# First MLP layer of an attention-MLP kernel: two of three token chunks by Strassen's algorithm in six of eight weight blocks

## The chip, the core and the metric

The kernel runs on one core of a Trainium2 chip. The metric is the device time of one execution in microseconds (us). Engines are called PE (TensorE matmul; PEld is its weight load), DVE (VectorE), ACT (ScalarE), POOL (GpSimd) and SP (SyncE, which here issues all DMAs). Each engine runs its own instruction stream in order; they meet only at semaphores.

## What is computed

The reference, cut to what matters here:

```python
x = attention(q, k, v, proj)        # 2 x 8 heads, 768 tokens, 64 wide -> x: 1536 x 512
h = x @ moe_w_in                    # 512 x 2048
r = np.maximum(h, 0.0)
g = s * (r * r) + b
y = g @ moe_w_out                   # 2048 x 512
a, c = y @ w1, y @ w2               # 512 x 1024 each
out = ((a * c) @ w3) @ w_out        # 1024 x 1024, 1024 x 512
```

All of it is float32. Each matmul factor is split into a high and a low part in a reduced format (`fp32r`), and a product is three matmuls: high by low, low by high, high by high.

## The kernel before, in words

Attention comes first; beside it `w3 @ w_out` is formed (`wc`). The stage that the change touches follows. Tokens are held transposed: `x_hi`, `x_lo` are 128 partitions x 4 row tiles (`KT`) x 1536 tokens, in three chunks of 512. The hidden width of 2048 goes in eight blocks (`fc`) of 256 = two tiles of 128. For a block and a chunk, PE forms two hidden tiles of 12 matmuls each (`hidden`, L1027, banks 0/1 or 2/3 in turn), and later four output tiles of 6 matmuls each (`out_of_hidden`, L1041, banks 4 to 7). PE takes the hidden tiles one chunk ahead of the outputs (`steps`, L1054). A waiting output product holds up all that stands behind it in PE's stream.

Between the two, ACT copies relu of the hidden tile out of PSUM (L637); DVE squares it with PSUM as the one operand (L847), scales it to `g_raw` (L851); ACT rounds it to `g_hi` (L643); DVE subtracts to `g_lo` (L855), and adds finished output tiles to `y_acc` (L867). DVE's order per step is: hidden work of the next chunk, then the four additions of this one (`steps`, L875).

Weights: SP loads 512 KB tiles into the two slots of `stage` (`load_w`, L253), and may issue tile w only when the low part of tile w-2 is done. ACT makes the high part (`w_high`, L556, in L558), POOL the low part (`w_low`, L406, in L408). A block has two tiles (`w_in`, `w_out`), in `w_c` or `w_b` by turns. The eight `w12` tiles of the next layer (`w1`, `w2`) go four into `w_a` in the first steps (`W12_A`), two into `w_c` in the last block and two into `w_b` behind the last output (`W12_B`, L681). The eight `wc_hi`/`wc_lo` splits (L630, L497) are made in steps 2 to 5 of the first six.

At the end `y_acc` is split for the next layer: ACT makes `x_hi` (L676), DVE `x_lo` (`y_low`, L869, in L873), chunk by chunk. The next layer (`second`, L1070) wants `x_lo` of chunk 0 to start; from its third unit of 24 matmuls on it also wants DVE's product `ab` (L896) of two units before, which needs ACT's copy `a_sb` (L690). In ACT's stream this copy stands behind the last `w12` high and the last `x_lo` (L683). Its last product with `wc` is L1095.

What orders the output products:

```python
def load_w(w, slot, src):
    after(sp, w_lo_done, w - 1)
...
pe.wait_ge(g_lo_done, 2 * n + 2)
for m in range(KT):
    after(pe, y_add_done, 4 * n + m - 3)
```

Of the kernel before, what the change touches and what calls it, by code (L numbers as in the profile page):

```python
# [41 lines left out]
def attention_mlp(nc, qk, v, proj, w_in, w_out, s, b, w12, w3t, w_out2, out):  # L42
    with ExitStack() as ctx:
# [171 lines left out]
        def _(sp):  # L215
# [291 lines left out]
        def _(act):  # L507
# [124 lines left out]
            def hidden(n, k):  # L632
                for f in range(2):

                    act.wait_ge(h_done, 2 * n + f + 1)
                    after(act, relu2_done, 2 * n + f - 1)
                    act.activation(relu[:, f], psum[:, 2 * (k % 2) + f, :], ACT.Relu).then_inc(relu_done, 1)  # L637
                for f in range(2):
# [4 lines left out]
                    act.activation(g_hi[:, k % 2, f], g_raw[:, f], ACT.Copy).then_inc(g_hi_done, 1)  # L643

            def steps(cp, first=False, last=False):
                for k in range(6):
                    hidden(6 * cp + k, k)
                    if k == 0:

                        after(act, y_mm_done, 24 * cp)  # L650
                        first_layer_weights(of_layer(2 * cp + 1), cp + 8 if first else 2 * cp + 10, 1)
                    if first and k in (1, 2):

                        for j in (2 * k - 2, 2 * k - 1):
                            w_high(W12_A + j, (W12_A + j) // 2 + 1, j % 2, high(w_a, j))
                    if first and k in (2, 3):
                        for i in range(4 * k - 8, 4 * k - 4):
                            wc_high(i)
                    if k == 3 and not last:
                        act.wait_ge(y_mm_done, 24 * cp + 12)  # L660
                        first_layer_weights(of_layer(2 * cp + 2), 2 * cp + 11, 0)
                    if k == 4 and last:
                        act.wait_ge(y_mm_done, 24 * cp + 12)
                        for j in range(2):
                            w_high(W12_B + j, W12_B // 2 + 1, j, high(w_c, j))
# [40 lines left out]
        def _(dve):  # L706
# [137 lines left out]
            def hidden(n, k):  # L844
                for f in range(2):
                    dve.wait_ge(relu_done, 2 * n + f + 1)
                    dve.scalar_tensor_tensor(relu2[:, f], psum[:, 2 * (k % 2) + f, :], 0.0, relu[:, f],  # L847
# [5 lines left out]
                for f in range(2):
                    dve.wait_ge(g_hi_done, 2 * n + f + 1)
                    dve.tensor_tensor(g_lo[:, k % 2, f], g_raw[:, f], g_hi[:, k % 2, f].bitcast(F32),  # L855
                                      ALU.subtract).then_inc(g_lo_done, 1)

            def add_y(n, t, first=False):
                for m in range(KT):
# [15 lines left out]
            def steps(cp, first=False, last=False):  # L875
                for k in range(6):
                    if not (last and k == 5):
                        hidden(6 * cp + k + 1, k + 1)
                    add_y(6 * cp + k, k % NCH, first=first and k < NCH)
                    if last and k == 4:  # L880
                        y_low(0)

            hidden(0, 0)
            steps(0, first=True)
# [19 lines left out]
        def _(pe):  # L904
# [149 lines left out]
            def steps(cp, last=False):  # L1054
                for k in range(6):
                    if not (last and k == 5):
                        hidden(6 * cp + k + 1, k + 1, 2 * cp + (k + 1) // NCH)
# [88 lines left out]
```

## Time and profile before

| what | value |
|---|---|
| median of 3 runs | 759.41 us (758.84 to 760.13) |
| the profiled execution | 759.74 us, span 758.0 us |
| mean granted TensorE clock | 0.999 |
| busy: PE, DVE, ACT, POOL | 733.6, 460.8, 375.8, 243.9 us |
| matmuls | 3848 |

The span runs from the first to the last instruction of the trace; the rest of an execution's time lies around it. Times in rows are us from the span's start unless marked ns. Matmuls are pipelined, so the duration of one (about 389 ns at 512 columns) is longer than its distance from the next; the distance is what a stream of them costs. The durations of DVE and POOL instructions include the time that an instruction waits after it was started.

### The profile page before, as it was taken

What the parts mean: (1) busy time and instruction counts of PE and PEld (TensorE: products, weight loads), DVE (VectorE), ACT (ScalarE), POOL (GpSimd) and SP (SyncE); (2) the same over time, 40 slices, a digit from 0 to 9 for tenths busy, and PEclk for the clock granted to TensorE, in tenths of its full rate; (3) what the DMA queues carried; (4) which work ended last, traced back from release to release, by engine and by line L of the source; (5) the groups of instructions that cost most, each with busy time, mean ns of one, the idle gap of its engine ahead of it and who ended that gap; (6) DMA issues with size and microseconds to landing.
All of it is one profiled execution on the core that took longest, in us unless ns stands there. A gap on an engine that the chain in (4) does not pass through costs nothing.

```text
span 758.0 us, 11068 instructions
## 1 busy us (share of the span) xinstructions
PE 733.6 (97%) x3848; PEld 634.5 (84%) x3848; DVE 460.8 (61%) x803; ACT 375.8 (50%) x701; POOL 243.9 (32%) x156
## 2 busy tenths in 40 slices
PE   2899999999999999999999999999999999999998
PEld 2778999999999988888888888888887888888886
DVE  4888989898899983776756576566593202210220
ACT  2798988989899984552322323132342211211220
POOL 4476656666665643591202012020220000000000
PEclk9999999999999999999999999999999999999999
DMA  5654443434443121311101011010100010000001
GB/s 139 158 154 117 105 116 78 106 79 124 105 106 87 36 97 59 117 59 56 56 1 55 1 55 40 16 55 1 56 0 1 1 42 15 1 28 28 0 0 55
DMA packets 17692, 45.55 MB, mean 60 GB/s; under 512 B 4946, under 2 KB 6994, under 8 KB 17650
## 3 DMA queue, kind: packets, MB, share of 16 engines
q1 hardware_dynamic: 17650, 44.99, 21.1%
q8 instruction: 26, 0.43, 0.2%
q14 instruction: 16, 0.13, 0.1%
HBM read 37.75 MB, written 3.19 MB: 54 GB/s over the span
## 4 chain that ended last, share of the span: by engine, by line
PE 92%; DVE 3%; DMA 2%; issue 1%; ACT 1%; SPq 1%; DVEq 0%; ACTq 0%
PE psum L1023 50%; PE psum L1095 9%; PE psum L950 8%; PE psum L937 8%; PE psum L968 5%; PE psum L926 4%; PE psum L920 4%; DVE x_lo L873 1%; DMA km<-qm 1%; PE psum L908 1%; DMA raw<-in_qk 1%; PE psum L911 1%; PE psum L910 1%; PE psum L909 1%; DVE top L753 1%
## 5 line engine op out<-in xcount | busy, mean ns | idle before, releaser
L767 DVE TENSOR_TENSOR pt_lo<-psum,pt_hi 128x384 fp32r<-128x384 f32 x192 | 97.7, 550 | 14.0 <-ACT pt_hi L545 13.3
L529 ACT ACTIVATE prob<-psum,exp_at 128x768 f32<-128x768 f32 x96 | 96.5, 1005 | 9.1 <-DVE exp_at L760 7.9
L753 DVE TENSOR_REDUCE top<-psum 128x1 f32<-128x768 f32 x96 | 90.9, 947 | 3.8 <-PE psum L926 3.7
L545 ACT ACTIVATE pt_hi<-psum 128x384 fp32r<-128x384 f32 x192 | 84.3, 494 | 17.4 <-PE psum L937 16.3
L637 ACT ACTIVATE relu<-psum 128x512 f32<-128x512 f32 x48 | 28.7, 598 | 127.6 <-PE psum L1023 127.6
L1023 PE MATMUL psum<-x_hi,w_c 128*128 128x512 f32 (+1 forms) x288 | 88.7, 389 | 0.0
L1023 PE MATMUL psum<-x_hi,w_b 128*128 128x512 f32 (+1 forms) x288 | 88.7, 389 | 0.0
L896 DVE TENSOR_TENSOR ab<-psum,a_sb 128x512 f32<-128x512 f32 x24 | 16.6, 691 | 117.8 <-ACT a_sb L690 117.8
L847 DVE SCALAR_TENSOR_TENSOR relu<-psum,relu 128x512 f32<-128x512 f32 x48 | 33.1, 689 | 83.0 <-ACT relu L637 83.0
L937 PE MATMUL psum<-ident,prob 128*128 128x128 f32 x576 | 80.0, 275 | 1.4 <-DVE pt_lo L767 0.9
L408 POOL TENSOR_TENSOR w_b<-stage,w_b 128x1024 fp32r<-128x1024 f32 x18 | 43.7, 2428 | 110.4 <-ACT w_b L558 109.2
L937 PEld LDWEIGHTS psum<-ident,prob 128*128 128x128 f32 x576 | 69.1, 142 | 6.9 <-issue 3.1
L950 PE MATMUL psum<-pt_hi,vs 128*128 128x384 f32 x192 | 65.1, 339 | 2.7 <-DVE o_sum L789 1.7
L950 PE MATMUL psum<-pt_lo,vs 128*128 128x384 f32 x192 | 64.6, 337 | 0.0
L1023 PEld LDWEIGHTS psum<-x_hi,w_c 128*128 128x128 f32 x288 | 54.0, 188 | 11.2
L1023 PEld LDWEIGHTS psum<-x_hi,w_b 128*128 128x128 f32 x288 | 54.0, 188 | 11.2
L920 PE MATMUL psum<-both_hi 128*128 128x512 f32 x192 | 58.1, 384 | 1.1 <-ACT prob L529 1.1
L1023 PE MATMUL psum<-g_hi,w_c 128*128 128x512 f32 x192 | 59.1, 389 | 0.0
L1023 PE MATMUL psum<-g_hi,w_b 128*128 128x512 f32 x192 | 59.1, 389 | 0.0
L1023 PE MATMUL psum<-x_hi,w_a 128*128 (+1 forms) x192 | 59.1, 389 | 0.0
L867 DVE TENSOR_TENSOR y_acc<-psum,y_acc 128x512 f32<-128x512 f32 x84 | 53.9, 684 | 6.2 <-PE psum L1023 5.8
L1023 PE MATMUL psum<-x_lo,w_c 128*128 128x512 f32 (+1 forms) x144 | 56.1, 390 | 0.0
(100 smaller groups left out, 1499.3 us busy)
## 6 DMA issues: line engine op xcount, KB each, us to landing
raw<-in_qk SPq DMA_DIRECT2D x30, 384.0 KB, 5.1
stage<-in_w_out SPq DMA_DIRECT2D x12, 512.0 KB, 3.3
stage<-in_w3t SPq DMA_DIRECT2D x8, 512.0 KB, 3.5
stage<-in_w_in SPq DMA_DIRECT2D x8, 512.0 KB, 3.3
stage<-in_w SPq DMA_DIRECT2D x8, 512.0 KB, 3.3
raw_v<-in_v SPq DMA_DIRECT2D x16, 192.0 KB, 2.8
qm<-both_hi SPq DMA_DIRECT2D x16, 192.0 KB, 2.7
r_sb<-r_rows SPq DMA_DIRECT2D x16, 192.0 KB, 5.4
```

The source lines that it names most:

```text
L408: pool.tensor_tensor(lo, stage[:, slot, :], hi.bitcast(F32), ALU.subtract).then_inc(w_lo_done, 1)
L529: act.activation(prob[:, t % 3], score[t % 2], ACT.Exp, bias=exp_at[:, t % 2, 1:2], scale=exp_at[:, t % 2, 0:1], accum_out=rsum[:, (t // 6 ...
L545: act.activation(pt_hi[:, u % 2, 3 * part:3 * part + 3, (t % 3) * P:(t % 3 + 1) * P], turned[part].rearrange("p (j q) -> p j q", j=3), ACT ...
L753: dve.tensor_reduce(top[:, t % 2, 1:2], score[t % 2], AX.X, ALU.max, negate=True).then_inc(top_done, 1)
L767: dve.tensor_tensor(pt_lo[at], turned[part].rearrange("p (j q) -> p j q", j=3), pt_hi[at].bitcast(F32), ALU.subtract).then_inc(pt_lo_done, 1)
L867: dve.tensor_tensor(at, psum[:, 4 + m, :], at, ALU.add).then_inc(y_add_done, 1)
L920: pe.matmul(score[t % 2][:, at], both_hi[:, par, 0, q], both_hi[:, par, 1, at], start=True, stop=False)
L937: tr = pe.transpose(turned[part][:, j * P:(j + 1) * P], prob[:, t % 3, blk * P:(blk + 1) * P], ident[:, :])
L950: mm = pe.matmul(o_ps, vs[:, (unit // 2) % 2, j], part[:, unit % 2, j], start=(j == 0 and part is pt_hi), stop=(j == TILES - 1 and part is ...
L968: mm = pe.matmul(wc_ps, terms[i][0], terms[i][1], start=(i == 0), stop=(i == len(terms) - 1))
L1023: mm = pe.matmul(psum[:, bank, :], lhs, rhs, start=(i == 0), stop=(i == len(terms) - 1))
L1095: mm = pe.matmul(psum[:, 4 + k, :], p[:, f, rows], w[:, f], start=(f == 0 and i == 0), stop=(f == FT - 1 and i == 2))
```

## The change

Blocks 0 and 1 stay as they were. In blocks 2 to 7 the hidden tiles of chunks 1 and 2 (the code's numbers; 0 is the first) are a 2 x 2 product of blocks: weights A (two column tiles by two halves of the depth) and tokens X (two halves of the depth by two chunks). Each of the eight block products was 6 matmuls. They become seven, M1 to M7, in Winograd's form: four sums S of A (POOL, from the raw weight in `stage`, each block) and four sums T of X (DVE, ten instructions of 1024 columns, once, in steps 0 to 3 of the first six), all split into high and low, and seven sums of the results on DVE, which lead to the four hidden tiles C11, C12, C21, C22 in SBUF (`work`). DVE squares these from SBUF (`chunk_of_pair`). PE's banks 0 to 3 serve M1 to M7.

The T splits occupy `w_a`, so that no `w12` tile can be loaded there during the blocks. All eight are now loaded behind them: two highs in the last block, two behind the split of y's chunk 0, two behind that of chunk 2, two at the end. The `wc` splits move to the last block. POOL now waits for its own instruction before each next one, and for the block before the last before it takes the next block's weights (`next_weights`). The diff, cut to its core and moved left by eight columns:

```diff
+    t_raw = sb("t_raw", [P, 4, 2, CHUNK], F32, before_split)
...
-    relu2 = sb("relu2", [P, 2, CHUNK], F32, c)
-    g_raw = sb("g_raw", [P, 2, CHUNK], F32, c)
+    work = sb("work", [P, 4, CHUNK], F32, c)
...
-w12_at = [(w_a, j) for j in range(4)] + [(w_c, 0), (w_c, 1), (w_b, 0), (w_b, 1)]
+w12_at = [(w_c, 0), (w_c, 1)] + [(w_a, j) for j in range(4)] + [(w_b, 0), (w_b, 1)]
...
+t_hi, t_lo = [w_a[:, k * 4 * WCH:(k + 1) * 4 * WCH].rearrange("p (i k n) -> p i k n", i=4, k=2)
+              for k in range(2)]
...
+FIRST7 = 2
+M1, M6, M5, M4, M7, M2, M3 = range(1, 8)
+U2, U3, C22, U4, C21, C11, C12 = range(1, 8)
+BANK_Y, BANK_X, BANK_Z, BANK_W = range(4)
+PAIR_TILES = ((0, 3), (2, 1))
+def products(fc, which):
+    return 7 * fc - 7 * FIRST7 + which
+def sums(fc, which):
+    return 7 * fc - 7 * FIRST7 + which
...
     load_w(of_layer(1) + 1, 1, w_out[1])
-    for k in range(4):
-        load_w(W12_A + k, k % 2, w12[k])
     with sp.Fori(2, NFC) as fc:
         load_w(of_layer(fc), 0, rows_of_chunk(w_in, fc))
         load_w(of_layer(fc) + 1, 1, rows_of_chunk(w_out, fc))
-    for k in range(4):
-        load_w(W12_B + k, k % 2, w12[4 + k])
+    for k in range(8):
+        load_w(W12 + k, k % 2, w12[k])
...
+    def s_sums(fc, par):
...
+        pool.wait_ge(staged[0], 16 * fc + 16 * (W_LAYER // 2 + 1))
+        pool.tensor_tensor(s1, a21, a22, ALU.add).then_inc(s_sum_done, 1)
+        pool.wait_ge(s_sum_done, done + 1)
+        pool.tensor_tensor(s2, s1, a11, ALU.subtract).then_inc(s_sum_done, 1)
+        pool.wait_ge(s_sum_done, done + 2)
+        pool.tensor_tensor(s3, a11, a21, ALU.subtract).then_inc(s_sum_done, 1)
+        pool.wait_ge(s_sum_done, done + 3)
+        pool.tensor_tensor(s4, a12, s2, ALU.subtract).then_inc(s_sum_done, 1)
+        pool.wait_ge(s_sum_done, done + 4)
+    def s_low(fc, par):
+        pool.wait_ge(s_hi_done, fc - FIRST7 + 1)
+        pool.tensor_tensor(s_lo[:, par], s_raw[:, par], s_hi[:, par].bitcast(F32),
+                           ALU.subtract).then_inc(s_lo_done, 1)
+        pool.wait_ge(s_lo_done, fc - FIRST7 + 1)
     pool.wait_ge(x_lo_done, PAIRS)
     w_low(of_layer(0) + 1, high(w_c, 1), low(w_c, 1), 1)
     pool.wait_ge(w_lo_done, of_layer(0) + 2)
-    first_layer_weights(of_layer(1), 1)
-    for k in range(4):
-        w_low(W12_A + k, high(w_a, k), low(w_a, k), k % 2)
+    layer_weights(1, 1)
+    s_sums(2, 0)
+    layer_weights(2, 0)
+    pool.wait_ge(t_sum_done, 10)
+    for i in range(4):
+        pool.wait_ge(t_hi_done, i + 1)
+        pool.tensor_tensor(t_lo[:, i], t_raw[:, i], t_hi[:, i].bitcast(F32), ALU.subtract).then_inc(t_lo_done, 1)
+        pool.wait_ge(t_lo_done, i + 1)
+    s_low(2, 0)
+    def next_weights(fc, par):
+        pool.wait_ge(y_mm_done, 12 * fc - 12)
+        s_sums(fc, par)
+        layer_weights(fc, par)
+        s_low(fc, par)
+    with pool.Fori(1, NFC // 2 - 1) as cp:
+        next_weights(2 * cp + 1, 1)
+        next_weights(2 * cp + 2, 0)
+    next_weights(NFC - 1, 1)
     for i in range(FT):
         pool.wait_ge(wc_hi_done, i + 1)
         pool.tensor_tensor(wc_lo[:, i], wc_raw[:, i], wc_hi[:, i].bitcast(F32),
                            ALU.subtract).then_inc(wc_lo_done, 1)
-    with pool.Fori(1, NFC // 2) as cp:
-        first_layer_weights(of_layer(2 * cp), 0)
-        first_layer_weights(of_layer(2 * cp + 1), 1)
-    for k in range(4):
-        w_low(W12_B + k, high(*w12_at[4 + k]), low(*w12_at[4 + k]), k % 2)
+        pool.wait_ge(wc_lo_done, i + 1)
+    for k in range(8):
+        w_low(W12 + k, high(*w12_at[k]), low(*w12_at[k]), k % 2)
+        pool.wait_ge(w_lo_done, W12 + k + 1)
...
+    def t_high(i):
+        act.wait_ge(t_sum_done, (3, 5, 8, 10)[i])
+        act.activation(t_hi[:, i], t_raw[:, i], ACT.Copy).then_inc(t_hi_done, 1)
...
+    def chunk0(fc, par):
+        relus(3 * fc, 2 * fc + 4 * FIRST7, 0)
+        g_highs(3 * fc, 3 * par, (0, 1))
+    def m1_copy(fc):
+        act.wait_ge(m_done, products(fc, M1))
+        act.activation(relu[:, 0], psum[:, BANK_X, :], ACT.Copy).then_inc(m1_copied, 1)
+    def chunks12(fc, par):
+        for c in range(2):
+            g_highs(3 * fc + 1 + c, 3 * par + 1 + c, PAIR_TILES[c])
+    for k in range(6):
+        relus(k, 2 * k, k)
+        g_highs(k, k, (0, 1))
+        if k == 0:
+            layer_weights(1, 1)
+        if k == 3:
+            act.wait_ge(y_mm_done, 12)
+            layer_weights(2, 0)
+        if k in (2, 3):
+            t_high(k - 2)
+        if k == 4:
+            t_high(2)
+            t_high(3)
+        if k == 5:
+            s_high(2, 0)
+    chunk0(2, 0)
+    def group(fc, par, last=False):
+        m1_copy(fc)
+        act.wait_ge(y_mm_done, 12 * fc)
+        if last:
+            w12_high(0)
+            w12_high(1)
+        else:
+            layer_weights(fc + 1, 1 - par)
+            s_high(fc + 1, 1 - par)
+        chunks12(fc, par)
+        if not last:
+            chunk0(fc + 1, 1 - par)
+    def y_high(t):
         act.wait_ge(y_add_done, 4 * (3 * NFC - NCH + t + 1))
...
+    with act.Fori(1, NFC // 2 - 1) as cp:
+        group(2 * cp, 0)
+        group(2 * cp + 1, 1)
+    group(NFC - 2, 0)
+    for i in range(FT):
+        wc_high(i)
+    group(NFC - 1, 1, last=True)
+    y_high(0)
+    act.wait_ge(m_done, products(NFC - 1, M3))
+    for k in range(2, 4):
+        w12_high(k)
+    y_high(1)
+    y_high(2)
+    for k in range(4, 6):
+        w12_high(k)
     act.wait_ge(y_mm_done, 12 * NFC)
-    for k in range(2):
-        w_high(W12_B + 2 + k, W12_B // 2 + 2, k, high(w_b, k))
+    for k in range(6, 8):
+        w12_high(k)
     act.wait_ge(y_lo_done, KT * NCH)
...
+    def g_of(tile):
+        dve.tensor_scalar(work[:, tile], work[:, tile], sb_col[:, 0:1], sb_col[:, 1:2],
+                          ALU.mult, ALU.add).then_inc(g_done, 1)
...
+    def combine(fc, which, out, bank, held):
+        dve.tensor_tensor(out, psum[:, bank, :], held, ALU.add).then_inc(combined, 1)
+        dve.wait_ge(combined, sums(fc, which))
+    def chunk_of_pair(fc, par, c):
+        n = 3 * fc + 1 + c
+        for f, tile in enumerate(PAIR_TILES[c]):
+            dve.scalar_tensor_tensor(work[:, tile], work[:, tile], 0.0, work[:, tile],
+                                     ALU.max, ALU.mult).then_inc(relu2_done, 1)
+            dve.wait_ge(relu2_done, 2 * n + f + 1)
+            g_of(tile)
+        g_lows(n, par + 1 + c, PAIR_TILES[c])
+    def t_sum(i, a, b, op, count):
+        dve.tensor_tensor(t_raw[:, i], a, b, op).then_inc(t_sum_done, 1)
+        dve.wait_ge(t_sum_done, count)
...
+    def t_sums(step):
+        t1, t2, t3, t4 = (t_raw[:, i] for i in range(4))
+        if step == 0:
+            dve.wait_ge(wc_mm_done, HEADS - 1)
+            t_sum(0, x_part(x_hi, 0, 2), x_part(x_hi, 0, 1), ALU.subtract, 1)
+            t_sum(0, t1, x_part(x_lo, 0, 2), ALU.add, 2)
+            t_sum(0, t1, x_part(x_lo, 0, 1), ALU.subtract, 3)
+        if step == 1:
+            t_sum(1, x_part(x_hi, 1, 2), t1, ALU.subtract, 4)
+            t_sum(1, t2, x_part(x_lo, 1, 2), ALU.add, 5)
+        if step == 2:
+            t_sum(2, x_part(x_hi, 1, 2), x_part(x_hi, 0, 2), ALU.subtract, 6)
+            t_sum(2, t3, x_part(x_lo, 1, 2), ALU.add, 7)
...
+    def group(fc, par, last=False):
+        n = 3 * fc
+        dve.wait_ge(m1_copied, fc - FIRST7 + 1)
+        dve.wait_ge(g_lo_done, 6 * fc + 2)
+        dve.wait_ge(m_done, products(fc, M6))
+        m1, u2, u3 = relu[:, 0], work[:, 2], work[:, 3]
+        combine(fc, U2, u2, BANK_Y, m1)
+        add_y(n, 0, which=range(2))
+        dve.wait_ge(m_done, products(fc, M7))
+        combine(fc, U3, u3, BANK_Y, u2)
+        combine(fc, C22, work[:, 1], BANK_Z, u3)
+        combine(fc, U4, u2, BANK_Z, u2)
+        combine(fc, C21, u3, BANK_W, u3)
+        dve.wait_ge(m_done, products(fc, M2))
+        combine(fc, C11, work[:, 0], BANK_X, m1)
+        chunk_of_pair(fc, par, 0)
+        add_y(n, 0, which=range(2, 4))
+        dve.wait_ge(m_done, products(fc, M3))
+        combine(fc, C12, u2, BANK_Z, u2)
+        chunk_of_pair(fc, par, 1)
+        add_y(n + 1, 1)
+        if last:
+            y_low(0)
+        else:
+            chunk0(fc + 1, 1 - par)
+        add_y(n + 2, 2)
     with dve.Fori(1, NFC // 2 - 1) as cp:
-        steps(cp)
-    steps(NFC // 2 - 1, last=True)
+        group(2 * cp, 0)
+        group(2 * cp + 1, 1)
+    group(NFC - 2, 0)
+    group(NFC - 1, 1, last=True)
...
+    def part(bank, w, x):
+        terms = [(w[a][:, j], x[b][:, j]) for j in range(2) for a, b in ((0, 1), (1, 0), (0, 0))]
+        for i, (lhs, rhs) in enumerate(terms):
+            mm = pe.matmul(psum[:, bank, :], lhs, rhs, start=(i == 0), stop=(i == len(terms) - 1))
+        mm.then_inc(m_done, 1)
+    def group(fc, par, last=False):
+        n, k = 3 * fc, 3 * par
...
+        pe.wait_ge(relu2_done, 2 * n + 2)
+        part(BANK_X, a(0, 0), x(0, 0))
+        pe.wait_ge(s_lo_done, fc - FIRST7 + 1)
+        part(BANK_Y, s(2), t(2))
+        part(BANK_Z, s(1), t(1))
+        part(BANK_W, a(1, 1), t(4))
+        out_of_hidden(n, k, fc, par, which=range(2))
+        pe.wait_ge(combined, sums(fc, U2))
+        part(BANK_Y, s(3), t(3))
+        pe.wait_ge(m1_copied, fc - FIRST7 + 1)
+        part(BANK_X, a(0, 1), x(1, 0))
+        out_of_hidden(n, k, fc, par, which=range(2, 4))
+        pe.wait_ge(combined, sums(fc, U4))
+        part(BANK_Z, s(4), x(1, 1))
+        if not last:
+            pe.wait_ge(combined, sums(fc, C11))
+            hidden(n + 3, 0, fc + 1, 1 - par)
+        out_of_hidden(n + 1, k + 1, fc, par)
+        out_of_hidden(n + 2, k + 2, fc, par)
+    pe.wait_ge(t_lo_done, 4)
     with pe.Fori(1, NFC // 2 - 1) as cp:
-        steps(cp)
-    steps(NFC // 2 - 1, last=True)
+        group(2 * cp, 0)
+        group(2 * cp + 1, 1)
+    group(NFC - 2, 0)
+    group(NFC - 1, 1, last=True)
...
-            if first and f in (4, 6):
-                pe.wait_ge(w_lo_done, W12_B + f - 2)
+            if first and f % 2 == 0:
+                pe.wait_ge(w_lo_done, W12 + f + 2)
```

## Rows read from the trace of the kernel before

**Rows 1.** The profile's busy times, whole span.

```profile
PE 733.6 (97%) x3848; PEld 634.5 (84%) x3848; DVE 460.8 (61%) x803; ACT 375.8 (50%) x701; POOL 243.9 (32%) x156
```

**Rows 2.** The chain that ended last, from 440 us: start, us, what.

```profile
439.98 118.11 PE psum L1023 x521
...
561.73 6.32 DVE x_lo L873 x3
...
568.07 0.61 ACT a_sb L690
...
568.70 0.70 DVE ab L896
...
569.45 32.94 PE psum L1023 x144
...
624.14 43.52 PE psum L1023 x192
```

**Rows 3.** Busy time by stretch: first steps after entry, blocks 2 to 5.

```profile
core 0: us, PE busy (x) PEld busy (x) DVE busy (x) ACT busy (x) POOL busy (x), PEclk, DMA share, GB/s
307.60:367.50 59.90, 59.90 (x266) 49.59 (x265) 44.75 (x59) 23.94 (x37) 28.95 (x16) 1.00 0.21 71
367.50:498.00 130.50, 130.50 (x577) 108.07 (x576) 81.79 (x120) 36.73 (x56) 19.19 (x8) 1.00 0.10 33
```

**Rows 4.** Instruction groups: shapes, count, busy us, mean ns, idle before.

```profile
L867 DVE TENSOR_TENSOR y_acc<-psum,y_acc 128x512 f32<-128x512 f32 x84 | 53.9, 684 | 6.2 <-PE psum L1023 5.8
```

**Rows 5.** DVE's timeline without POOL beside it: start, us, instruction.

```profile
303.06 0.69 DVE L847 SCALAR_TENSOR_TENSOR relu<-psum,relu 128x512 f32<-128x512 f32 x1 [1.34 <-ACT relu L637]
303.79 0.55 DVE L851 TENSOR_SCALAR g_raw<-relu,sb_col 128x512 f32<-128x512 f32 x1
304.25 1.48 DVE L855 TENSOR_TENSOR g_lo<-g_raw,g_hi 128x512 fp32r<-128x512 f32 x2
```

**Rows 6.** The timelines of DVE and POOL, 336 to 344 us.

```profile
338.42 0.69 DVE L847 SCALAR_TENSOR_TENSOR relu<-psum,relu 128x512 f32<-128x512 f32 x1 [0.73 <-ACT relu L637]
339.15 2.44 DVE L851 TENSOR_SCALAR g_raw<-relu,sb_col 128x512 f32<-128x512 f32 x1
341.51 0.68 DVE L847 SCALAR_TENSOR_TENSOR relu<-psum,relu 128x512 f32<-128x512 f32 x1
342.23 1.92 DVE L851 TENSOR_SCALAR g_raw<-relu,sb_col 128x512 f32<-128x512 f32 x1
...
336.41 2.54 POOL L497 TENSOR_TENSOR wc_lo<-wc_raw,wc_hi 128x512 fp32r<-128x512 f32 x2
338.91 2.40 POOL L408 TENSOR_TENSOR w_c<-stage,w_c 128x1024 fp32r<-128x1024 f32 x1
341.47 2.40 POOL L408 TENSOR_TENSOR w_c<-stage,w_c 128x1024 fp32r<-128x1024 f32 x1 [0.16 <-POOL w_c L408]
```

**Rows 7.** `x_lo` instructions alone (to 561.7 us) and later; POOL's timeline there.

```profile
L873 DVE TENSOR_TENSOR x_lo<-y_acc,x_hi x5: 683/684/684, 558.7 to 561.1; 128x512 fp32r<-128x512 f32 x5
...
L873 DVE TENSOR_TENSOR x_lo<-y_acc,x_hi x3: 686/2884/2898, 561.7 to 565.1; 128x512 fp32r<-128x512 f32 x3
...
562.13 5.36 POOL L408 TENSOR_TENSOR w_b<-stage,w_b 128x1024 fp32r<-128x1024 f32 x2 [17.23 <-ACT w_b L558]
```

**Rows 8.** ACT's timeline behind the last output.

```profile
558.84 2.19 ACT L676 ACTIVATE x_hi<-y_acc 128x512 fp32r<-128x512 f32 x4 [3.25 <-DVE y_acc L867]
560.94 2.00 ACT L558 ACTIVATE w_b<-stage 128x1024 fp32r<-128x1024 f32 x2
```

**Rows 9.** DMA issues, 300 to 560 us: count, size, us to landing.

```profile
stage<-in_w SPq DMA_DIRECT2D x8, 512.0 KB, 3.3
```

**Rows 10.** Matmuls of L909 (384 columns), 9 to 26.6 us and later.

```profile
L909 PE MATMUL psum<-both_hi,pw x3: 522/522/522, 10.2 to 25.1; 128*128 128x384 f32 x3
...
L909 PE MATMUL psum<-both_hi,pw x29: 332/332/341, 27.9 to 261.7; 128*128 128x384 f32 x29
...
L908 PE MATMUL psum<-both_hi,pw 128*128 128x384 f32 x3 | 1.9, 622 | 10.9 <-DVE km L714 9.7 <-DVE qm L746 1.2
```

More of the change, by code:

```diff
@@ L642, in hidden @@
                         after(act, y_mm_done, 4 * n - 4)
[L643 to L665, printed above, removed]
@@ L667, in _ @@
-            steps(0, first=True)
-            with act.Fori(1, NFC // 2 - 1) as cp:
-                steps(cp)
-            steps(NFC // 2 - 1, last=True)
-            for t in range(NCH):
+                    act.activation(g_hi[:, k % 2, f], work[:, tiles[f]], ACT.Copy).then_inc(g_hi_done, 1)
+            def chunk0(fc, par):
[4 more added lines that the diff above has]
+                act.activation(relu[:, 0], psum[:, BANK_X, :], ACT.Copy).then_inc(m1_copied, 1)
@@ L848, in hidden @@
+            def hidden(n, h, k, par):
+                for f in range(2):
+                    dve.wait_ge(relu_done, h + f + 1)
+                    after(dve, g_lo_done, 2 * n + f - 1)
+                    dve.scalar_tensor_tensor(work[:, f], psum[:, 2 * (k % 2) + f, :], 0.0, relu[:, f],
                                              ALU.max, ALU.mult).then_inc(relu2_done, 1)
                     dve.wait_ge(relu2_done, 2 * n + f + 1)
-                    dve.tensor_scalar(g_raw[:, f], relu2[:, f], sb_col[:, 0:1], sb_col[:, 1:2],
-                                      ALU.mult, ALU.add).then_inc(g_done, 1)
@@ L853, in hidden, with chunk0 @@
[L853 to L859, printed above, removed]
+                    g_of(f)
+                g_lows(n, par, (0, 1))
+            def chunk0(fc, par):
+                hidden(3 * fc, 2 * fc + 4 * FIRST7, 0, par)
@@ L860, in add_y @@
+            def add_y(n, t, first=False, which=range(KT)):
+                for m in which:
                     dve.wait_ge(y_mm_done, 4 * n + m + 1)
@@ L873, in y_low @@
                     dve.tensor_tensor(x_lo[at], y_acc[at], x_hi[at].bitcast(F32), ALU.subtract).then_inc(y_lo_done, 1)
[L875 to L884, printed above, removed]
+            hidden(0, 0, 0, 0)
+            for k in range(6):
+                hidden(k + 1, 2 * k + 2, k + 1, k + 1)
+                add_y(k, k % NCH, first=k < NCH)
+                t_sums(k)
+            def group(fc, par, last=False):
[24 more added lines that the diff above has]
+                add_y(n + 2, 2)
             with dve.Fori(1, NFC // 2 - 1) as cp:
-                steps(cp)
-            steps(NFC // 2 - 1, last=True)
+                group(2 * cp, 0)
+                group(2 * cp + 1, 1)
+            group(NFC - 2, 0)
+            group(NFC - 1, 1, last=True)
             for t in range(1, NCH):
@@ L1024, in product, with hidden @@
                 return mm
-            def hidden(n, k, fc):
-                par = (k // NCH) % 2
+            def hidden(n, k, fc, par):
                 at = slice((k % NCH) * CHUNK, (k % NCH + 1) * CHUNK)
@@ L1039, in hidden, with out_of_hidden @@
                             ).then_inc(h_done, 1)
-            def out_of_hidden(n, k, fc):
-                par = (k // NCH) % 2
+            def out_of_hidden(n, k, fc, par, which=range(KT)):
                 if k % NCH == 0:
@@ L1045, in out_of_hidden @@
                 pe.wait_ge(g_lo_done, 2 * n + 2)
-                for m in range(KT):
+                for m in which:
                     after(pe, y_add_done, 4 * n + m - 3)
@@ L1052, in out_of_hidden @@
                             ).then_inc(y_mm_done, 1)
[L1054 to L1057, printed above, removed]
-                    out_of_hidden(6 * cp + k, k, 2 * cp + k // NCH)
             pe.wait_ge(x_lo_done, PAIRS)
-            hidden(0, 0, 0)
+            hidden(0, 0, 0, 0)
             pe.wait_ge(wc_raw_done, HEADS - 1)
-            steps(0)
+            for k in range(6):
+                hidden(k + 1, k + 1, (k + 1) // NCH, ((k + 1) // NCH) % 2)
+                out_of_hidden(k, k, k // NCH, k // NCH)
```

67 lines of the change are left out of this document (53 added, 14 removed).

## The prediction

> **What bounds the kernel now.** I read the busy times first. PE is busy 97% of the span [rows 1], so only shortening PE's stream, or opening a gap in it, moves the end. The chain of waits says the same: from 440 to 558 us it is PE's stream alone, and only behind it does it leave PE, for 11 us of DVE's splitting of the accumulated activations (`x_lo`), one ACT copy and one DVE product, then PE again to the end [rows 2]. In the changed stage PE has no gap: 264 matmuls fill 307.6 to 367.5 us, and the four middle blocks run the same way [rows 3]. One 512-column matmul takes 43.52/192 = 0.2267 us of that stream [rows 2]. There DVE is busy 82 of 130 us and POOL 19; this slack is what the change spends.
>
> **What it saves.** Six blocks lose one product of 6 matmuls each: 36 x 0.2267 = 8.16 us, all on the path. A block is now 138 matmuls, 31.28 us.
>
> **What it adds off PE.** DVE gets seven sums a block, each from PSUM and SBUF like the 0.684 us additions [rows 4]; each waits for the one before, and such a dependent pair starts 0.73 apart [rows 5]. Ten T sums of 1024 columns run once: no such row exists. Bounds are 0.7 (the 512-column row) and 2 x 0.68 = 1.4; I take 1.22, from the 512-column 0.684 with a small fixed part and one column a ns. POOL gets four S sums a block (256 columns; the 512-column one takes 1.27, half of the pair in [rows 6]; bounds 0.6 and 1.27, taken 0.74), a 2.4 us split of S, and once four T splits of 2.4. ACT loses four relu copies a block and gains two copies: free, since it works 37 of 130 us [rows 3]. The M1 copy and S splits are ready more than 5 us before use. The weight DMAs are the same number; those for the next stage all move behind the blocks.
>
> **The rule that decides.** A DVE instruction that reads only SBUF and a POOL instruction exclude each other. DVE's 0.55 us `g` took 2.44 and 1.92 when a 2.40 POOL split ran, while its PSUM-reading neighbours kept 0.69 [rows 5, 6]. The `x_lo` splits took 0.68 each alone (minimum, median and largest of five), and two took 2.9 beside POOL's two splits at 562 us [rows 7]: one POOL instruction passes before each. Whether the squares, now also from SBUF alone, obey this no row shows; a two-input subtraction from SBUF is nearest and obeys, so I take it; if not, 0.7 us less in the last block. The Trainium skill (SBUF — State Buffer, Who interferes with whom) says that a DVE instruction with two SBUF inputs contends with a GpSimd one that reads SBUF; by it the 0.7 is paid.
>
> **Steady blocks: no stall.** From a block's start, PE runs M1, M6, M5, M4, two output products, M7 (8.16 to 9.7), M2, two more outputs, M3 (13.6 to 14.96), next block's chunk 0 (to 20.4), then outputs of chunks 1 and 2. POOL's work (3.0 + 4.8 + 2.4) ends at 10.5, before DVE's SBUF work begins. DVE makes its five sums from 9.7 to 13.3 and the first square ends at 14.0; PE wants it at 14.96: margin 0.9. `g_lo` of chunk 1 is ready at 17.2 for 20.4: margin 3.2; of chunk 2, and the additions, 2.3. All thin, all positive.
>
> **Place 1, the sixth chunk: 3.4 us.** In steps 2 and 3 DVE takes T sums after its additions. Two of step 2's three each wait for a weight split, so the next chunk's first square moves from 338.4 [rows 6] to 344.0; with 3.8 of that chunk, 2.4 of additions and 2.5 of T sums the tenth sum ends at 352.7. Only there may POOL start its four T splits and the S split, 12 us of 2.40 without a pause. They meet the sixth chunk's second `g` (wait 1.8) and both `g_lo` (2.5 each): the first addition behind ends at 365.4. PE wants it 5.44 before 367.5 [rows 3], at 362.1.
>
> **Place 2, the last block: 3.3 + 0.9 us.** It has no next chunk 0, so the 5.44 us of cover is gone. From M7's start PE is ready for chunk 1's output at 6.80 (30 matmuls). DVE: M7 ends 1.52, five sums 3.62, squares and `g` 0.72 + 0.47 + 0.72 + 0.47, `g_lo` 0.79 + 0.72: 9.05. POOL is there in a row: the eight `wc_lo`, moved here from the first steps, and then two weight splits; the first square waits 1.05 more. 10.1 - 6.8 = 3.3. Chunk 2 then waits for 0.87: DVE has two additions, one sum, squares and splits to do, 6.3 us from the last `g_lo` to the end of the first addition, against 5.44 of PE.
>
> **Place 3, entry of the next layer: 3.7 us.** PE ends the last output 5.44 after its start, at 557.3; the next layer wants `x_lo` of chunk 0. DVE begins those four after the additions, at 553.5, just as ACT hands POOL the third and fourth `w12` tile, which came earlier before. Two of the four wait 2.48 each [rows 7]: 561.0.
>
> **Place 4, behind it: 6.3 us.** Before, two tiles were left behind the last addition: ACT spent 2.2 and 2.0 [rows 8], and PE, 48 matmuls into the layer from 557.9, waited from 568.8 to 569.45 [rows 2]. Now four are left and the stage buffer holds two. Last addition 563.4; ACT's four `x_hi` 2.1 and two `w12` highs to 567.4; POOL's split of the fifth tile 566.97 to 569.4; of the sixth, after an `x_lo`, to 572.5; only then is the eighth tile's DMA issued, 3.3 to land [rows 9], 575.8; ACT's high 1.0; and behind these stands, in ACT's queue, the first `a_sb`: 576.8, then 0.6 and DVE's product 0.7: 578.2. PE has done two units (10.9) at 571.9 and needs the buffer.
>
> **Sum.** 3.4 + 3.3 + 0.9 + 3.7 + 6.3 = 17.6, less 0.7 that PE waits there already, less 8.2: +8.7. The profiled execution took 759.74 (span 758.0): 768.4.
>
> **The clock.** A 384-column matmul took 522 ns up to 25.1 us and 332 from 27.9 [rows 10], a start-to-start of 320 ns being 1.2 GHz; PE had idled 9.7 us before its first. (The granted-clock column says 1.00 in both stretches, so matmul durations are to be read.) No later gap in the trace comes near 6.3 us. Bounds after such a gap: nothing, and 3.0 us, half of the 5.9 us from 20.8 to 26.7 in which PE was nearly always busy and still slow. I take 2.3, by the gap-free part (22.0 to 26.7). A drop in place 3 costs nothing: it shortens the wait in place 4. Total 770.7; the median of the runs shown is 0.33 below the profiled one: **770.4**.
>
> **Rivals.**
> - *A, the gain comes whole, 751.3*: waits at the four places are covered. For it: PE is by far the busiest and DVE's idle share is 39%. Against: at each place the wait is a chain with no idle time in it. The Trainium skill (Perfetto Trace Analysis, Identifying the Most-Contended Engine) says to optimise the engine of highest occupancy first, which is what this does; by it the time falls. Chance 0.07.
> - *B, DVE and POOL get past each other* where the new instructions meet. Then place 1 and 3 vanish, place 2 is 2.2 + 0.9, place 4 is 4.0: 7.1 - 8.2 = -1.0, about 758.4, no change. Against: [rows 7]. Chance 0.04.
> - *C, the steady blocks stall too.* If each sum takes 0.2 us more than taken, the square misses chunk 0 by 0.3 in five blocks and place 2 grows by 1.3: 773; at 0.5 more, 788. It decides from 0.15 us a sum. For it: margin 0.9. Against: 84 additions of this form average 684 ns. Chance 0.11.
> - *D, the product isn't saved* (PE still issues it): the waits alone, 778.6. The diff's M1 to M7 are 42 matmuls against 48. Chance 0.02.
> - Forecast as summed: 0.76.
>
> The forecast's own range is 764 (no clock drop, DMA and locks kinder by 4 in all) to 774. With part of C: 764 to 775. A measurement of this kernel tells 0.2%, 1.5 us, from no change. Faster is A: 0.07; same B with a bit of the forecast's edge: 0.05; slower 0.88.
>
> **What would show it.** PE's matmuls 3812. Waits of PE: on DVE's addition or `g_lo` near 362 us and 542 us, on `x_lo` near 557, on `ab` near 572; none between 370 and 540. `x_lo` instructions of 3 us beside POOL. An ACT `a_sb` that waits for the last stage DMA. Matmuls at 0.43 us spacing behind the long wait. Wrong if PE never waits over 1 us at these places, or if the blocks' period isn't 31.3 us.

## The result, and the profile after

The changed kernel takes 768.77 us (median of 4 runs, 768.22 to 770.02), the one before 759.18 on the same chip: a ratio of 1.0129, 95% interval 1.0116 to 1.0141, so 9.6 us slower. The profiled execution took 770.02 and is the slowest of the four; its span is 768.2 against 758.0.

The profile's busy times and the granted clock in its 40 slices, kernel after:

```profile
PE 730.8 (95%) x3812; PEld 631.6 (82%) x3812; DVE 496.1 (65%) x855; ACT 374.1 (49%) x693; POOL 290.2 (38%) x190
...
PEclk9999999999999999999999999999998999999999
```

3812 matmuls are 36 fewer than in [rows 1]: the products are gone. Yet the span is 10.2 us longer, and a slice near 580 us has a lower clock. All of it arises in the changed stage and behind it: the layer's first product starts at 296.46 us (296.62 before), and from there to the end it is 471.8 us against 461.4. DVE has 35 us more work, POOL 46; over the whole span neither is near its limit (65% and 38% busy). What PE waited for from 296 us on (us in total, times, longest), kernel after:

```profile
PE psum L1217 <- DVE ab L1090: 6.5, 1, 6.5
PE psum L1217 <- DVE g_lo L970: 4.0, 1, 4.0
PE psum L1217 <- issue: 2.2, 1, 2.2
PE psum L1217 <- DVE y_acc L1036: 1.8, 1, 1.8
```

Four waits, one each: 14.5 us. Before there was one of 0.5. These are times in which PE shows no work; where this text speaks of a gap it means the distance of two matmul starts beyond the usual 0.23 us, which is 0.1 to 0.2 longer. By stretch, in the columns of [rows 3], kernel after (the first steps of the stage; blocks 2 to 6; the last block; the next layer's first chunk):

```profile
307.00:367.00 60.00, 58.15 (x257) 47.83 (x256) 55.59 (x63) 19.79 (x30) 27.22 (x13) 1.00 0.11 36
...
371.90:527.00 155.10, 155.10 (x686) 128.44 (x686) 115.70 (x185) 42.86 (x65) 50.64 (x35) 1.00 0.10 34
527.00:558.00 31.00, 26.64 (x110) 21.26 (x108) 24.41 (x31) 12.47 (x20) 18.33 (x11) 0.94 0.14 47
558.00:624.00 66.00, 57.67 (x243) 47.25 (x244) 20.43 (x30) 16.85 (x26) 11.43 (x5) 0.95 0.09 31
```

Blocks 2 to 6 run without a gap (155.10 of 155.10). The loss is in front of them and behind, and behind them the granted clock is 0.94 and 0.95 on average.

**The four places, read in the timelines.** Start, us, instruction; what ended the idle time before stands in brackets. Place 1, DVE, then POOL:

```profile
354.92 0.68 DVE L978 SCALAR_TENSOR_TENSOR work<-psum,relu 128x512 f32<-128x512 f32 x1
355.64 1.90 DVE L964 TENSOR_SCALAR work<-work,sb_col 128x512 f32<-128x512 f32 x1
357.47 5.67 DVE L970 TENSOR_TENSOR g_lo<-work,g_hi 128x512 fp32r<-128x512 f32 x2
...
352.20 10.40 POOL L551 TENSOR_TENSOR w_a<-t_raw,w_a 128x1024 fp32r<-128x1024 f32 x4 [9.88 <-issue]
362.67 2.72 POOL L538 TENSOR_TENSOR s_lo<-s_raw,s_hi 128x1024 fp32r<-128x1024 f32 x1
```

The T splits stand in one row, as forecast; the pair of `g_lo` that takes 1.48 alone takes 5.67. PE was ready at 361.9. Place 2, DVE, then POOL:

```profile
538.47 0.69 DVE L989 TENSOR_TENSOR work<-psum,relu 128x512 f32<-128x512 f32 x1
539.19 2.55 DVE L995 SCALAR_TENSOR_TENSOR work<-work 128x512 f32<-128x512 f32 x1
...
536.26 4.93 POOL L437 TENSOR_TENSOR w_c<-stage,w_c 128x1024 fp32r<-128x1024 f32 x2
```

The first square of C11 takes 2.55 beside a weight split, the others of this block 0.69. Place 3, DVE, then POOL:

```profile
552.88 6.88 DVE L1042 TENSOR_TENSOR x_lo<-y_acc,x_hi 128x512 fp32r<-128x512 f32 x4
559.69 2.47 DVE L1036 TENSOR_TENSOR y_acc<-psum,y_acc 128x512 f32<-128x512 f32 x4
...
553.05 5.57 POOL L437 TENSOR_TENSOR w_a<-stage,w_a 128x1024 fp32r<-128x1024 f32 x2 [11.86 <-ACT w_a L629]
```

PE's first matmul of the next layer starts at 559.87; the view of waits puts this wait down to "issue", but DVE's last `x_lo` of chunk 0 ends at 559.76. Place 4, ACT, then PE:

```profile
562.19 2.20 ACT L777 ACTIVATE x_hi<-y_acc 128x512 fp32r<-128x512 f32 x4 [6.28 <-DVE y_acc L1036]
564.29 2.00 ACT L629 ACTIVATE w_a<-stage 128x1024 fp32r<-128x1024 f32 x2
572.43 1.06 ACT L629 ACTIVATE w_b<-stage 128x1024 fp32r<-128x1024 f32 x1 [6.13 <-DMA stage<-in_w]
575.17 1.06 ACT L629 ACTIVATE w_b<-stage 128x1024 fp32r<-128x1024 f32 x1 [1.68 <-DMA stage<-in_w]
576.13 0.58 ACT L809 ACTIVATE a_sb<-psum 128x512 f32<-128x512 f32 x1
...
577.49 0.79 PE L1217 MATMUL psum<-x_lo,w_a 128*128 128x512 f32 x1 [6.46 <-DVE ab L1090]
578.08 1.05 PE L1217 MATMUL psum<-x_hi,w_a 128*128 128x512 f32 x2
```

ACT stands 7.8 us before stage DMAs (6.13 and 1.68) while a finished product of PE waits for the copy `a_sb`. And the pair of matmuls behind PE's wait takes 1.05 where such pairs take 0.62: the granted clock from 577.5 to 582 us is 0.50, the lower of its two levels (1.2 GHz). Below, slow matmuls are those behind a gap that start more than 0.35 us after the one before; most of them stand 0.43 apart, where 0.23 is usual.

### The profile page after: what moved, and what is told of

Same layout as the page of the kernel before. It is cut to its first block, busy times and chain, and to the rows that moved or that the text cites. A ratio compares the mean times of both kernels' runs of the same rounds, so it can differ in the third digit from the quotient of the medians.

```text
span 768.2 us, 11189 instructions
## 1 busy us (share of the span) xinstructions
PE 730.8 (95%) x3812; PEld 631.6 (82%) x3812; DVE 496.1 (65%) x855; ACT 374.1 (49%) x693; POOL 290.2 (38%) x190
## 4 chain that ended last, share of the span: by engine, by line
PE 83%; DVE 7%; issue 3%; ACT 2%; DMA 2%; POOL 1%; SPq 0%; DVEq 0%; POOLq 0%; ACTq 0%
PE psum L1217 36%; PE psum L1329 8%; PE psum L1144 8%; PE psum L1131 7%; PE psum L1258 7%; PE psum L1162 5%; PE psum L1120 4%; PE psum L1114 4%; DVE t_raw L1003 1%; DMA km<-qm 1%; DVE y_acc L1036 1%; DVE top L872 1%; DMA raw<-in_qk 1%; PE psum L1102 1%; POOL w_a L437 1%
## 5 line engine op out<-in xcount | busy, mean ns | idle before, releaser
L727 ACT ACTIVATE g_hi<-work 128x512 fp32r<-128x512 f32 x48 | 30.4, 632 | 134.3 <-DVE work L964 134.3
L1217 PE MATMUL psum<-x_hi,w_c 128*128 128x512 f32 (+1 forms) x192 | 59.2, 389 | 0.0
L1217 PE MATMUL psum<-x_hi,w_b 128*128 128x512 f32 (+1 forms) x192 | 59.1, 389 | 0.0
L1120 PE MATMUL psum<-km,qm 82*128 82x512 f32 x192 | 50.8, 347 | 4.7 <-DMA km<-qm 4.7
L809 ACT ACTIVATE a_sb<-psum 128x512 f32<-128x512 f32 x24 | 14.3, 596 | 80.2 <-PE psum L1217 80.2
L1162 PE MATMUL psum<-w_a,w_b 128*128 128x256 f32 x336 | 49.9, 285 | 0.0
L1162 PEld LDWEIGHTS psum<-w_a,w_b 128*128 128x128 f32 x336 | 43.8, 189 | 2.6
```

Source lines behind the costliest of these rows:

```text
L1120: mm = pe.matmul(score[t % 2][:, at], qm[0:82, par, q], km[0:82, par, at], start=False, stop=True)
L1162: mm = pe.matmul(wc_ps, terms[i][0], terms[i][1], start=(i == 0), stop=(i == len(terms) - 1))
L1217: mm = pe.matmul(psum[:, bank, :], lhs, rhs, start=(i == 0), stop=(i == len(terms) - 1))
```

## The experiments

All edit the changed kernel. Medians are compared with the kernel before on the same chip (759.25 for e1 to e4, 758.76 for e5 and e6, 759.05 for e7 and e8). The part of a profiled execution ahead of the changed stage is the same program in all, but not the same time: the layer's first product starts at 294.93 to 296.54 us in the changed kernel and e1 to e4. So the profiles are also compared by the time from that product to the end, called the rest: 471.8 us in the changed kernel.

**e1: the last two `w12` highs out of the way of `a_sb`.**

```diff
-            act.wait_ge(y_mm_done, 12 * NFC)
-            for k in range(6, 8):
-                w12_high(k)
...
                     act.activation(ab_hi[:, f], ab[:, f % 2], ACT.Copy).then_inc(ab_hi_done, 1)
+                    if first and f == 1:
+                        for k in range(6, 8):
+                            w12_high(k)
```

> The changed kernel with one edit in ACT's stream: the highs of the last two w12 tiles stand behind the second unit of the next layer (after its ab_hi), not ahead of the first a_sb. Theory (the wait of 6.6 us at 571 us is the chain addition, x_hi, w12 highs, POOL splits, stage DMA, w12 highs, a_sb): a_sb is then held by the last x_lo alone (567 us), 1.5 us before PE needs the product at 570.9, so the wait goes, and with it the 11 matmuls at 0.43 us pitch behind it: 768.8 - 6.6 - 2.4 = 759.8, between 759 and 761. Rival (PE waits there because DVE's x_lo splits and POOL's splits exclude each other, whatever stands in ACT's queue): the wait stays, 768 to 769.

Measured: 761.47 (ratio to the kernel before 1.0030, 1.0018 to 1.0041); 7.3 us off for one move in one queue. PE's waits, e1:

```profile
PE psum L1216 <- DVE g_lo L969: 4.0, 1, 4.0
PE psum L1216 <- DVE y_acc L1035: 1.8, 1, 1.8
PE psum L1216 <- issue: 1.4, 1, 1.4
```

The wait for `ab` is gone, and ACT copies `a_sb` at 565.77, long before PE asks. The rival falls. The median is 0.5 above the range. The profiled execution, 759.73, was the fastest of the ten and started the layer 1.5 us earlier than the changed kernel's; its rest is 463.0, 8.7 less. What the slower executions lost no trace shows; behind the 4.2 us gap that remains 13 matmuls were slow here, 7 in the changed kernel's profile, so this differs from run to run.

**e2: the T splits as their sums are done.**

```diff
+            t_low(0, 4, 1)
             layer_weights(2, 0)
-            pool.wait_ge(t_sum_done, 10)
-            for i in range(4):
...
+            t_low(2, 8, 2)
+            t_low(1, 9, 3)
+            t_low(3, 10, 4)
```

> The changed kernel with POOL's T splits begun when their own sums are done (order T1 ahead of the third block's weight splits, then T3, T2, T4) in place of all four behind the tenth sum. Theory (the 2.1 us wait at 362 us is POOL's unbroken row of T splits passing ahead of DVE's g and g_lo of the sixth chunk): wait under 0.5 us, 766.9, between 766.3 and 767.5. Rival (the T sums themselves make DVE late, POOL or not): the wait stays at 2 us, 768.8.

Measured: 767.77 (1.0115, 1.0097 to 1.0133). In time this can't be told from the changed kernel, but the trace decides it. PE's waits, e2:

```profile
PE psum L1222 <- DVE ab L1095: 6.5, 1, 6.5
PE psum L1222 <- DVE g_lo L975: 4.0, 1, 4.0
PE psum L1222 <- issue: 1.4, 1, 1.4
```

No wait near 362 us: DVE still makes all ten T sums, so it was the unbroken row. The saved 2.0 us shows in the profile, whose rest is 469.3, 2.5 less (place 3 is 0.8 shorter too, and 21 matmuls are slow against 18). The medians show only 1.0 and miss the expected range by 0.3; four executions each, which scatter by 1.7 and 1.8 us, can't tell the two apart.

**e3: the `wc` splits out of the last block.** ACT's `wc_high` and POOL's eight splits moved behind the `w12` tiles, into the next layer's first chunk; PE waits for each of them at its first use.

```diff
             group(NFC - 2, 0)
-            for i in range(FT):
-                wc_high(i)
             group(NFC - 1, 1, last=True)
...
+                    if first and f == 2:
+                        for i in range(FT):
+                            wc_high(i)
```

> The changed kernel with the wc splits (ACT's eight highs, POOL's eight lows) moved from the last block into the first chunk of the next layer. Theory (in the last block 1.9 of the 4.1 us wait at 540.8 us is the square that lay behind a POOL split, the rest is the missing cover): the wait falls to 2.3 us, the matmuls behind it stay at 0.23 us pitch, and the 0.9 us wait of chunk 2 comes back: 768.8 - 1.9 - 1.8 + 0.9 = 766.0, between 765 and 767.5. Rival 1 (exclusion costs nothing for squares from SBUF, the whole wait is DVE's chain): 768 to 769. Rival 2 (POOL's row was the whole wait): no wait at all there, 762.9.

Measured: 769.16 (1.0120, 1.0096 to 1.0144): no gain, a miss. The gap at place 2 was 2.29 as expected, the square ran undisturbed, and chunk 2's wait did not come back; e3, DVE:

```profile
540.10 0.69 DVE L990 TENSOR_TENSOR work<-psum,relu 128x512 f32<-128x512 f32 x1
540.83 0.69 DVE L996 SCALAR_TENSOR_TENSOR work<-work 128x512 f32<-128x512 f32 x1
```

So exclusion holds for squares from SBUF (2.55 against 0.69), and both rivals fall. In the profile the clock took the gain: the gaps are 1.7 us less in sum, but 8 matmuls were slow even behind the smaller gap, and 8 behind the 2.0 us gap of place 1, where the changed kernel's profile has none (last section); slow matmuls cost 1.8 us more in sum, and the rest is 471.9 against 471.8. Whether the other three executions, 767.14 to 770.22, lost it in the same way no trace shows.

**e4: `x_hi` of chunk 1 ahead of `w12` tiles 2 and 3.**

```diff
+            y_high(1)
             for k in range(2, 4):
                 w12_high(k)
-            y_high(1)
```

> The changed kernel with ACT's x_hi of chunk 1 put ahead of the highs of w12 tiles 2 and 3, so that POOL's two splits come after DVE's x_lo of chunk 0. Theory: the 2.4 us wait for x_lo at 557.5 goes, but the stage slots come free later, so the chain to the eighth tile ends no earlier and PE's wait at 571 grows by what is gained: 768 to 770, no change in sum. Rival (the places are independent, the gain stays): 766.4.

Measured: 768.42 (1.0125, 1.0107 to 1.0142). Place 3 has no gap any more. PE is ready for the product at 567.5 and waits 6.4 us, where it waited 6.6 before. PE's wait and DVE, e4, where the eight `x_lo` of chunks 1 and 2 took 4.89 before this edit:

```profile
PE psum L1217 <- DVE ab L1090: 6.3, 1, 6.3
...
552.16 2.48 DVE L1042 TENSOR_TENSOR x_lo<-y_acc,x_hi 128x512 fp32r<-128x512 f32 x4
...
557.39 12.04 DVE L1042 TENSOR_TENSOR x_lo<-y_acc,x_hi 128x512 fp32r<-128x512 f32 x8
```

The median is what the theory said, the trace is not: the wait at place 4 did not grow by the 2.4 us. The chain in front of it moved with place 3, since DVE adds chunk 2's outputs behind the `x_lo` of chunk 0: ACT copies the first `a_sb` at 572.54, at 576.13 in the changed kernel. The rest is 468.5, 3.3 less, and the profiled execution took 765.99, near the rival's 766.4. But it is the fastest of four; the others took 768.33 to 769.69 at a mean granted clock of 0.988 to 0.991 against 0.993, and have no trace. Whether the gain of place 3 stays is open.

**e5: 2.7 us more of PE's own work between M7 and chunk 1's output.**

```diff
-                out_of_hidden(n, k, fc, par, which=range(2))
+                if not last:
+                    out_of_hidden(n, k, fc, par, which=range(2))
...
-                out_of_hidden(n, k, fc, par, which=range(2, 4))
+                out_of_hidden(n, k, fc, par, which=range(4) if last else range(2, 4))
```

> The changed kernel with M7 and M2 of the last block put ahead of all four outputs of its chunk 0 (2.7 us more of PE's own work between M7 and the output of chunk 1), DVE's two additions moved behind with them. Theory (the wait at 540.8 us is DVE's chain of 10.9 us from M7's start against 6.8 us of PE's work, 9.5 now): wait 1.4 us and no slow matmuls behind it, but chunk 2's outputs then wait some 1 to 2 us as DVE has two more additions to do: 765 to 767. Rival (the wait is tied to POOL's row, not to M7): the wait at that place stays over 3 us and the time within 0.5 of 768.8.

Measured: 769.95 (1.0140, 1.0125 to 1.0154), a miss. The gap stayed at 4.26, as the rival said of the wait. DVE, e5, then POOL:

```profile
538.72 2.32 DVE L995 SCALAR_TENSOR_TENSOR work<-work 128x512 f32<-128x512 f32 x1
541.08 2.49 DVE L964 TENSOR_SCALAR work<-work,sb_col 128x512 f32<-128x512 f32 x1
...
538.09 5.20 POOL L437 TENSOR_TENSOR w_c<-stage,w_c 128x1024 fp32r<-128x1024 f32 x2
```

The chain of sums now starts 2.3 us nearer to POOL's row (3.0 us before the weight splits, 0.7 in the changed kernel) and meets two of them instead of one: 3.6 us lost, not 1.9. PE waits on the addition behind `g_lo` here (4.1). Gap and slow matmuls differ place by place (place 4 is 4.9 here), but the rest is 471.7, the changed kernel's. Cover and row depend on each other; one without the other shows little.

**e6: all five edits.**

> The five edits together. Theory (the four places are all that eats the saved 36 matmuls): waits of PE after 300 us under 1.5 us in sum, no matmuls at 0.43 us pitch after 30 us, 759.2 - 8.2 - 0.7 + 0 to 1.5 = 750.3 to 752. Rival (something in the steady blocks or in the sums costs as well and was covered by the waits): over 754.

Measured: 757.81 (0.9986, 0.9973 to 0.9999), 5.8 us above the range and in the rival's, over 754. Gaps: none at places 1 and 3, 0.7 and 1.3 in the last block, and a new one of 3.8 at 562.1 with 12 slow matmuls. e6, DVE, POOL, ACT:

```profile
552.02 12.47 DVE L1047 TENSOR_TENSOR x_lo<-y_acc,x_hi 128x512 fp32r<-128x512 f32 x8
...
550.71 5.23 POOL L437 TENSOR_TENSOR w_a<-stage,w_a 128x1024 fp32r<-128x1024 f32 x2 [19.07 <-ACT w_a L634]
557.71 5.64 POOL L437 TENSOR_TENSOR w_a<-stage,w_a 128x1024 fp32r<-128x1024 f32 x2 [1.76 <-ACT w_a L634]
...
564.53 0.60 ACT L808 ACTIVATE a_sb<-psum 128x512 f32<-128x512 f32 x1 [4.34 <-DVE x_lo L1047]
```

Four POOL splits passed among the eight `x_lo`, and ACT waits for the last `x_lo` before the first `a_sb`. The rival's cause falls nevertheless: PE is busy for all 155.10 us of the steady blocks here too.

**e7: e6, with tiles 4 and 5 moved too** (highs behind the first unit of the next layer, 6 and 7 behind the third, `wc` behind the fourth). The diff is against e6.

```diff
-            for k in range(4, 6):
-                w12_high(k)
...
-                    if first and f == 1:
-                        for k in range(6, 8):
+                    if first and f in (0, 2):
+                        for k in range(4 + f, 6 + f):
                             w12_high(k)
-                    if first and f == 2:
+                    if first and f == 3:
                         for i in range(FT):
```

> The five edits, and the highs of w12 tiles 4 and 5 also moved behind the first unit of the next layer (6 and 7 behind the third, the wc splits behind the fourth). Theory (in the five-edit kernel the 3.8 us wait at 562 us is a_sb behind the last x_lo, whose eight instructions were passed by four POOL splits): with two of the four gone x_lo ends near 559.5, before PE needs ab, so the wait and the 12 slow matmuls behind it go: 757.8 - 3.8 - 0.4 - 2.4 = 751.2, between 750.5 and 753. Rival (the x_lo splits take 12 us whatever POOL does): 757 to 758.

Measured: 752.48 (0.9914, 0.9901 to 0.9928), in the range. PE's one entry of waits for the stage, and its stretches, e7:

```profile
PE psum L1221 <- DVE y_acc L1039: 1.7, 2, 1.2
```

```profile
371.90:527.00 155.10, 155.10 (x686) 128.44 (x685) 115.47 (x184) 39.80 (x60) 47.91 (x31) 1.00 0.10 34
527.00:556.00 29.00, 27.29 (x120) 22.00 (x119) 24.28 (x37) 12.41 (x20) 8.66 (x4) 1.00 0.14 42
556.00:622.00 66.00, 66.00 (x293) 54.66 (x292) 19.78 (x23) 20.09 (x32) 22.20 (x13) 1.00 0.13 46
```

Same arithmetic and the same number of instructions on every engine as the changed kernel (3812 on PE, 855, 693 and 190 on DVE, ACT and POOL), 16.3 us less; no matmul is slow in this stretch. This beats both kernels: 6.6 us under the one before.

**e8: e7 with M5 formed twice in each block.** The diff is against e7.

```diff
+                for i, (p, q) in enumerate((p, q) for j in range(2) for p, q in ((0, 1), (1, 0), (0, 0))):
+                    pe.matmul(psum[:, BANK_Z, :], s(1)[p][:, i // 3], t(1)[q][:, i // 3], start=(i == 0), stop=(i == 5))
                 part(BANK_Z, s(1), t(1))
```

> The kernel of e7_tail_again with the product M5 of each of the six blocks formed twice (the first result is overwritten), so 36 matmuls are added. Theory (in the steady blocks PE's stream is all of the path): 36 x 0.2267 = 8.2 us more than e7, less up to 1.2 us of the waits left in the last block, since M5 there stands before DVE's chain: +7.5 to +8.2. Rival (DVE is close to the bound in the blocks, so part of the saved work is waited for elsewhere): +5 or less.

Measured: 760.38 (1.0016, 1.0008 to 1.0025), 7.9 over e7, in the range; the rest is 8.1 longer in the profiles. So the six products' 36 matmuls are worth some 8 us where nothing else is in the way: the saving is real and whole, the steady blocks included.

## Why the prediction was right, point by point

- **The saving**, 8.16: 7.9 by e8. And e7 against the kernel before is -6.6 in the medians (-6.8 in the rests); -8.2 and the 0.7 gap of before gone, against 2.0 of gaps left in the last block, is -6.9.
- **The prices without a row** were close: 1.22 taken for a T sum alone and 0.74 for an S sum, 1.22 and 0.74 measured.
- **Steady blocks without a stall**: shown, 155.10 of 155.10, with sums of 0.69 as in [rows 4]. Rival C falls.
- **The rule of exclusion** carried three of the four places, and the row that was missing is there now: 2.55 for a square from SBUF beside POOL, 0.69 alone. The Trainium skill (SBUF — State Buffer, Who interferes with whom) says that a DVE instruction with two SBUF inputs contends with a GpSimd instruction that reads SBUF; this trace agrees for the square. Rival B falls by e2 and e3.
- **Place 1**, forecast 3.4, measured 2.0. The mechanism held (e2), the term was mis-sized: the tenth T sum ended at 352.1, not 352.7; the second `g` waited 1.35, not 1.8; the two `g_lo` waited 4.2 in sum (5.67 less 1.48), not 5.0. With DVE's instructions between them four T splits took 10.40, 2.6 each.
- **Place 2**, forecast 3.3 + 0.9, measured 4.1 and no second wait. The square lay 1.9 behind POOL, not 1.05. The second wait, I think, was covered by something that I had priced only behind place 4: slow matmuls, which gave DVE 1.6 us. No run shows it by itself, but in e7, where none is slow, a second gap of 1.35 is there.
- **Place 3**, forecast 3.7, measured 2.4: PE came later, DVE on time. From M7's end to the last `x_lo` of chunk 0 I had 24.1 us; it took 24.2 (535.57 to 559.76). DVE never stood without work there, so it, not PE, sets the pace of the last block. In e3 the same stretch took 22.4: a shorter chain on DVE does bring the entry of the next layer forward.
- **Place 4**, forecast 6.3, measured 6.6. The mechanism is shown by e1.
- **The clock**: forecast 2.3 behind place 4; 11 slow matmuls cost 2.4. The forecast put the fall behind place 2 at nothing, and that failed: behind the 4.1 us gap 7 matmuls were slow and cost 1.6 us.
- **Sum**: gaps 2.0 + 4.1 + 2.4 + 6.6 and slow matmuls 1.6 + 2.4, less 0.7 and 8.2, is +10.2, against a rest that is 10.4 longer. Forecast +11.0, measured +9.6 in the medians. That the number is so near is luck in part: place 1, the second wait of place 2 and place 3 were 3.6 too much together, the first wait of place 2, place 4 and the unpriced slow matmuls 2.7 too little.
- **Rival A** would have been about right for e7's order of the queues (751.3 against 752.5), and was wrong for this one. The Trainium skill (Perfetto Trace Analysis, Identifying the Most-Contended Engine) says to optimise the engine of highest occupancy first; that was worth 6.6 us with e7's order and cost 9.6 with this one.
- **Two slips in the rivals' prices**: B leaves out the 0.7 that the forecast takes off, and C at 0.5 us a sum comes to some 784 by its own terms (six sums ahead of each square, 2.1 in each of five blocks, 3.3 at place 2), not 788. Both rivals fell on other grounds.

## What to carry to other kernels

Work taken off the busiest engine is gained only if every hand-over that the work covered still has cover: walk through the ends of the changed stage (first use, last block, entry of the next one), not only its steady part. Moving preparation "behind" a stage puts it into an in-order queue ahead of something that is needed at once; here two ACT instructions ahead of a copy cost 7.3 us. And when waits stand in a row, test the edits together as well as singly: in the medians e3, e4 and e5 gave nothing each, while with e1, e2 and one more move all gave 16.3. Together they cleared the places they were made for: in e7 the gap of 4.1 at place 2 is 0.7 and 1.35, and place 3 has none. How much of the 16.3 is theirs isn't measured, since no run has e1, e2 and the last move without them.

## What was not expected of the hardware

The clock falls after shorter gaps than I had thought, and not always. Read from matmul starts after 296 us in the profiles of the changed kernel and e1 to e6: behind the 11 gaps of 3.8 us or more 6 to 13 slow matmuls followed every time; behind nine gaps of 2.0 to 2.4 us three times (8, 8 and 9); behind gaps of 1.6 or less never. That last is no safe rule: in attention, where many matmuls are narrower, the granted clock fell near 50 us in five of the ten profiles (changed kernel, e3, e5, e7, e8; 0.61 to 0.63 on average over 49.6 to 54.0 us against 1.00 in the others), with no two matmul starts between 30 and 54 us more than 1.9 apart. The same stretch around place 1, with the same gap of 2.01, in the changed kernel and in e3 (columns as above):

```profile
361.00:369.00 8.00, 6.15 (x28) 4.78 (x27) 7.83 (x11) 1.86 (x3) 4.31 (x2) 1.00 0.00 0
```

```profile
361.00:369.00 8.00, 6.15 (x20) 4.63 (x20) 7.83 (x11) 1.86 (x3) 4.37 (x2) 0.79 0.00 0
```

28 matmuls against 20 in 8 us, clock 1.00 against 0.79, one and the same program there. The slow matmuls cost 1.6 us. Together with the 1.6 us by which the layer's start differs between the profiles of e1 to e4, this chance is as large as what e2 to e5 were to show, and four executions each are too few for such edits; its share in the untraced executions was not measured. Also, which of DVE and POOL goes first when both have instructions waiting isn't fixed: in the changed kernel eight `x_lo` ran unbroken in 4.89 us while a POOL split that had its start at 565.51 had to wait (two of the eight started after it), and in e4 and e6 four splits passed among the eight (12.04 and 12.47). What decides it, the runs leave open.
